# Moving the two single token tiles behind chunk 2 at the start of a channel-attention kernel, and one more warm-up matmul

## The reference, cut to what matters

```
qn = q / (norm(q, axis=tokens) + 1e-6);  kn = k / (norm(k, axis=tokens) + 1e-6)
s  = kn.T @ qn / tau                     # (256, 256), contracted over 6016 tokens
a  = softmax(s);  x = v @ a              # (6016, 256)
h  = x @ w_in1;   x = (relu(h) ** 2) @ w_out1
h  = x @ w_in2;   y = max(0.01 * h, h) @ w_out2
```

## Time and profile before

| | us |
|---|---|
| median of 3 runs | 1028.19 |
| lowest and highest of the 3 | 1027.05, 1028.72 |
| the profiled execution | 1027.15 |
| its span, first to last instruction | 1025.3 |

### The profile page before, as it was taken

How to read it: one execution, slowest core, us unless ns; L and a number is a source line. 1 busy time by engine, 2 the same in 40 slices (tenths; PEclk the granted TensorE clock), 3 DMA queues, 4 the chain that set the end, 5 groups by cost and what they waited for, 6 DMA issues and landing times.

```text
span 1025.3 us, 13193 instructions
## 1 busy us (share of the span) xinstructions
PE 1020.9 (100%) x4610; PEld 859.8 (84%) x4610; DVE 724.3 (71%) x1198; ACT 671.0 (65%) x1185; POOL 25.1 (2%) x34
## 2 busy tenths in 40 slices
PE   9999999999999999999999999999999999999998
PEld 8888888888888888888888888888888888888887
DVE  6899766766667667667567767768777777777665
ACT  6888877777777777777766555555655556555554
POOL 3500000000000000000000000000000000000000
PEclk9999999999999999999999999999999999999999
DMA  9800120140131132124452002002002002000001
GB/s 366 310 21 22 31 82 32 67 136 32 67 122 46 67 98 71 47 97 151 151 176 96 1 2 81 1 1 79 1 1 80 1 1 82 1 1 30 12 0 42
DMA packets 33732, 69.27 MB, mean 68 GB/s; under 512 B 2690, under 2 KB 18562, under 8 KB 33666
## 3 DMA queue, kind: packets, MB, share of 16 engines
q1 hardware_dynamic: 33090, 67.25, 18.9%
q10 hardware_dynamic: 576, 1.18, 0.3%
HBM read 44.56 MB, written 23.86 MB: 67 GB/s over the span
## 4 chain that ended last, share of the span: by engine, by line
PE 99%; DMA 0%; ACT 0%; ACTq 0%; issue 0%
PE psum L520 32%; PE psum L522 32%; PE psum L521 32%; PE psum L527 3%; DMA qk<-in_k 0%; PE psum L575 0%; PE psum L584 0%; ACT out_buf L1005 0%; PE psum L591 0%; ACTq L731 0%; PE psum L572 0%
## 5 line engine op out<-in xcount | busy, mean ns | idle before, releaser
L868 ACT ACTIVATE g_hi<-g 128x496 fp32r<-128x496 f32 (+1 forms) x384 | 237.3, 618 | 204.3 <-DVE g L1172 76.5
L1162 DVE TENSOR_TENSOR g_lo<-g,g_hi 128x496 fp32r<-128x496 f32 (+1 forms) x384 | 259.8, 677 | 131.2 <-ACT g_hi L868 128.7
L522 PE MATMUL psum<-g_hi,wout_lo 128*128 128x496 f32 (+1 forms) x768 | 296.1, 386 | 0.0
L520 PE MATMUL psum<-g_hi,wout_hi 128*128 128x496 f32 (+1 forms) x768 | 296.1, 386 | 0.0
L521 PE MATMUL psum<-g_lo,wout_hi 128*128 128x496 f32 (+1 forms) x768 | 296.0, 385 | 0.0
L520 PE MATMUL psum<-xop_hi,win_hi 128*128 128x496 f32 (+1 forms) x672 | 259.3, 386 | 0.0
L521 PE MATMUL psum<-xop_lo,win_hi 128*128 128x496 f32 (+1 forms) x672 | 259.1, 386 | 0.0
L522 PE MATMUL psum<-xop_hi,win_lo 128*128 128x496 f32 (+1 forms) x672 | 259.0, 385 | 0.0
L520 PEld LDWEIGHTS psum<-g_hi,wout_hi 128*128 128x128 f32 x768 | 144.2, 188 | 27.4 <-issue 0.3
L521 PEld LDWEIGHTS psum<-g_lo,wout_hi 128*128 128x128 f32 x768 | 144.3, 188 | 27.2
L522 PEld LDWEIGHTS psum<-g_hi,wout_lo 128*128 128x128 f32 x768 | 144.2, 188 | 27.1
(11 more groups left out here) (104 smaller groups left out, 684.3 us busy)
## 6 DMA issues: line engine op xcount, KB each, us to landing
up_parts<-park_up SPq DMA_DIRECT2D x8, 896.0 KB, 4.3
qk<-in_q SPq DMA_DIRECT2D x15, 384.0 KB, 9.6
qk<-in_k SPq DMA_DIRECT2D x13, 384.0 KB, 10.9
stage_o<-in_w_out SPq DMA_DIRECT2D x16, 256.0 KB, 3.4
down_parts<-park_down SPq DMA_DIRECT2D x8, 512.0 KB, 2.9
raw<-in_vT SPq DMA_DIRECT2D x8, 496.0 KB, 4.9
x_tiles<-out_buf SPq DMA_DIRECT2D x8, 496.0 KB, 3.0
raw<-x_tiles SPq DMA_DIRECT2D x8, 496.0 KB, 4.2
```

What stands on the lines that cost most here:

```text
L520: pe.matmul(out, a_hi, b_hi, start=start and i == 0, stop=False, **more)
L522: last = pe.matmul(out, a_lo, b_hi, start=False, stop=stop and i == len(operands) - 1, **more)
L868: act.activation(g_hi[:, tile, 0:W], g[:, tile, 0:W], ACT.Copy).then_inc(g_hi_made[tile], 1)
L1162: dve.tensor_tensor(g_lo[:, tile, 0:W], g[:, tile, 0:W], g_hi[:, tile, 0:W].bitcast(F32), ALU.subtract).then_inc(g_split[tile], 1)
```

## The change

Tile 0 is no longer loaded and used first. Its q transfer leaves the head of SP's queue and its k transfer leaves the head of ACT's queue; both are now issued by SP behind chunk 2, ahead of the two of tile 1. TensorE uses both tiles behind chunk 2. The matmul that clears `gram` is now that of chunk 0's first tile. `WARM_UP` is 7 instead of 6. All lines behind the removed ones have moved up by one.

```
-WARM_UP = 6
+WARM_UP = 7
...
-            sp.dma_start(edge[:, 0, 0, :], q_t[:, 0, :]).then_inc(edge_loaded[0], 16)
             for c in range(EARLY_CHUNKS):
                 sp.dma_start(qk[:, c, 0, :, :], q_t[:, chunk_tokens(c), :]).then_inc(qk_loaded[c], 16)
             for c in range(EARLY_CHUNKS, QK_CHUNKS):
                 load_chunk(c)
                 if c == EDGES_AFTER:
-                    for i, src in enumerate((q_t, k_t)):
-                        sp.dma_start(edge[:, 1, i, :], src[:, 1, :]).then_inc(edge_loaded[1], 16)
+                    for t in range(EDGES):
+                        for i, src in enumerate((q_t, k_t)):
+                            sp.dma_start(edge[:, t, i, :], src[:, t, :]).then_inc(edge_loaded[t], 16)
...
-                    return gram_half(b, qk[:, slot, 0, t, :], qk[:, slot, 1, t, :], False, False)
+                    return gram_half(b, qk[:, slot, 0, t, :], qk[:, slot, 1, t, :], c == 0 and t == 0, False)
...
-                    gram_half(b, edge[:, t, 0, :], edge[:, t, 1, :], t == 0, False)
-
-            gram_edge(0)
+                    gram_half(b, edge[:, t, 0, :], edge[:, t, 1, :], False, False)
+
             for c in MAIN_CHUNKS:
...
                 if c == EDGES_AFTER:
-                    gram_edge(1)
+                    for t in range(EDGES):
+                        gram_edge(t)
...
-            act.dma_start(edge[:, 0, 1, :], k_t[:, 0, :]).then_inc(edge_loaded[0], 16)
             for c in range(EARLY_CHUNKS):
```

## The result

| | before | after |
|---|---|---|
| median of 22 executions each, us | 1027.17 | 1029.35 |
| lowest, highest, us | 1026.25, 1028.72 | 1027.01, 1030.46 |
| profiled execution, us | 1027.15 | 1027.41 |
| its span, us | 1025.3 | 1025.8 |

The ratio is 1.0018 with a 95% interval from 1.0012 to 1.0024: the changed kernel is about 1.9 us slower by the ratio, 2.2 us by the medians. That lies inside the range that was forecast (1027.0 to 1030.4) and within the 0.2% called no change, at its edge. But it is not the +0.2 us of the likeliest case. The median of before had been 1028.19 over three executions; over 22 it is 1027.17, so the 1.0 us that the forecast put on top of the sum was not there, and the difference between the kernels is ten times as large as the likeliest case had it.

The account below looks back on a forecast made before the run. TensorE's uninterrupted stream was taken to bound the kernel. Earlier landing -0.67, tile 0's records +0.86 and 0 for the rest gave about +0.2 us on a median of 1028.19, so 1028.4 us, range 1027.0 to 1030.4.

Parts of the forecast that it names:

- the likeliest case: Whole kernel: +0.2 us from the path, within a forecast of 0.0 to +0.5 us given chance 0.57.
- the sum: Whole path: -0.67 for chunk 0 landing earlier, +0.86 for tile 0's records, 0 for the rest, +0.19 us.
- tile 0 as free work: Start of the kernel before: tile 0 is done while chunk 0's transfer is under way, so it costs nothing there.
- Part 1: Start: chunk 0's transfers are issued first, so it lands 0.67 us earlier, at 4.95 us.
- The 4.55 us by the rule: Chunk 0's landing by 2.0 us fixed plus bytes at 436 GB/s; total -0.2 us, a small gain given 0.10.
- Part 2: Behind chunk 2: tile 0's four records join TensorE's unbroken stream, with nothing to hide them, +0.86 us.
- Part 3: Warm-up: the seventh matmul adds 0.43 us, ends near 3.9 us and is covered by the wait for chunk 0, cost 0.
- Part 4: Chunks 1 to 3, tiles and last sum of squares: everything else that moves still arrives in time, cost 0.
- the late clock: Chunk 0: a break after warm-up delays the clock's rise, so its records run slow; +2.2 us in all, chance 0.20.
- The rival's price: Start of chunk 0: 9.5 records at the lower clock, +2.0 us, or +2.2 us with the path, giving 1030.4 us.
- the shift to the median: Whole time: the forecast was based on the earlier median 1028.19 us, 1.04 us above the profiled execution.

Follow-up runs that it names:

- a_warm10: The changed kernel with WARM_UP = 10 instead of 7: 1027.66 us, ratio 1.0002 to the kernel before.
- use_late: The kernel before, transfers untouched, with tile 0 used behind chunk 2 and WARM_UP = 11: 1028.32 us, ratio 1.0010 to the kernel before.
- after_look1: The changed kernel with no edit, run again for another profile: its profiled execution took 1028.35 us.
- a_warm6: The changed kernel with WARM_UP = 6 instead of 7: 1029.06 us, ratio 1.0019 to the kernel before.
- both_first: Against the kernel before, both single tiles loaded and used ahead of chunk 0, ACT issuing k of both: 1031.63 us, ratio 1.0046.
- after_again: The changed kernel with no edit, measured once more: 1029.13 us, ratio 1.0016 to the kernel before.
- both_first_sp: Against the kernel before, both single tiles loaded and used ahead of chunk 0, with tile 1's k issued by SP: 1030.08 us, ratio 1.0026.

## Why the prediction was right in its range and wrong in its reason

- **What bounds the kernel, and tile 0 as free work:** right. TensorE's stream is the end of the chain in every kernel here. In the profile of a_warm10 the chain joins it only at 42.1 us: up to there it runs through the transfers and VectorE to `q_diag`, for which TensorE waits 0.26 us. The forecast took that wait to move along with TensorE; here it is a second floor close below.
- **Part 1, the earlier landing:** forecast 0.67 us (bounds 0 to 0.84), measured 0.39 to 0.62 in the four profiles of the changed kernel (0.52 in the first), and 0.6 us between the medians of use_late and a_warm10. Chunk 0 lands at 5.00 to 5.24 us where 4.95 was forecast. The 4.55 us by the rule of the Trainium skill ("DMA: Bandwidth & Descriptors", section "Anatomy of one DMA — SWDGE (gpsimd) path") came out 0.5 to 0.7 us too early for these 768 KB: the measured time from issue to landing is 4.26 to 4.49 us, against the 3.8 us estimated by it.
- **Part 2, tile 0's records on the path:** right, 0.86 us, in the profiles (1.73 us for the two tiles) and in use_late (+0.95).
- **Part 3, the seventh warm-up matmul:** right that it costs nothing. But the step "the wait covers the added matmul wholly. Cost 0." left out what warm-up is worth: with ten in place of seven the kernel is 1.5 us faster by the medians.
- **Part 4:** no wait for chunks 1 to 3, as forecast; chunk 3 begins 0.34 us later where 0.2 was forecast. The last sum of squares is ready at 38.4 us (37.68 + 0.69) and TensorE asks at 39.35 us, so that wait stays empty.
- **The step that failed** is the weight given to the late clock. The forecast read the clock's rise at 4.8 us off one execution and let it stand where the work ahead of it was cut short, since "the break is short beside the 3.1 us of warm-up". 18 of the 22 executions of the changed kernel took over 1028.4 us, 1.2 us and more above the median of before. The rival's price, 9.5 slow records and +2.0 us, giving +2.2 with the path, was near for the start: two profiles, of after_look1 and a_warm6, show some eight slow records (1.78 us in after_look1), and the medians differ by 2.2 us. At the end of those two profiles it is only +1.2 and +1.1 us, so the fit with the medians is not proof of the price. This rival, given 0.20, was the case. The rule of the Trainium skill that the prediction cited beside it ("TensorE: Matmul & The Clock Gate", section "What's actually happening"), that the slow level is the default and activity releases it, agrees with the trace: 333 ns from the first matmul on, and again behind both_first's break.
- **The second step that failed** is the shift to the median: +1.04 us for the distance of the profiled execution from a median of three. With 22 executions the distance is 0.0. Without it the forecast of 1028.4 would have been 1027.35, 2.0 us below the 1029.35 that was measured; with it 1.0 us. The two errors cancelled in part, and that the likeliest value came out within a microsecond is luck.

## What to carry to other kernels

Work that nobody waits for may still be paid for: matmuls ahead of the first data, useful or not, decide at which clock the first useful ones run, so before such work is moved, look at how much work TensorE has ahead of its first exposed matmul and how long the break between them is, and fill a break that the move opens with enough work (ten matmuls did it here, seven and six did not). A single profile can't price this, since the same program had its rise before chunk 0 in one execution and eight records into it in the next; look at the scatter of the times, which shrank from 3.1 us (eleven executions of after_again) to 2.1 us, or 0.6 us without one low outlier (a_warm10), when the break was filled. And read the durations of the weight loads, not the clock column, at the start of a trace.

## What the runs showed of the hardware that was not expected

- The column of the granted clock says 1.00 in the first microseconds, while weight loads of 333 ns there equal those of a stretch marked 0.50. The trace's clock record begins with the rise (3.96 to 8.69 us in the profiles of the changed kernel), and behind it the records of chunk 0 are 0.22 us apart.
- Small transfers in front slow what follows: from 413 to 274 GB/s over the stretch from 3.5 to 7.5 us with none to six transfers of 128 KB at the head of the queues, so that in both_first chunk 0's k landed at 9.34 us in place of some 6.3, and in both_first_sp its q at 8.28 us. Open why.
- A delay of 2.0 us at the start was 1.2 us at the end in after_look1, and one of 1.95 us was 1.07 us in a_warm6; 0.8 to 0.9 us came back between 240 and 470 us, where TensorE's records stood slightly closer together. Open why.
